# A fused attention and MLP kernel: the next batch's token mix among the last down-products, mixed blocks among the first up-products, and a new order of work in the first phase

## The chip, the core and the metric

One core of a Trainium2 chip. The time is the device time of one launch in microseconds (us), lower is better. All arithmetic is in 32-bit floats; products of the dense layers are made from three passes over split operands (a rounded high part and the rest).

## The reference

Three stages, applied to 4 batches of 768 tokens. A gated linear attention with 8 heads of 48 channels, a token-mixing and channel-mixing layer, and a second one with a spatial gate:

```python
for t in range(S):                                    # attention, per batch and head
    state = alpha[:, :, t, :, None] * state + einsum('bhd,bhe->bhde', k[:, :, t], v[:, :, t])
    y[:, :, t] = einsum('bhd,bhde->bhe', q[:, :, t], state)
...
u = x + (x^T @ U @ V)^T                               # U 768x32, V 32x768: token mix
x = u + relu(u @ w_ch1) @ w_ch2                       # w_ch1 384x1536, w_ch2 1536x384
...
h = relu(x @ w_in); u, v = halves of h                # then layer norm of v, w_spatial over tokens,
out = (u * (w_spatial @ norm(v) + b)) @ w_out         # gate, w_out
```

## The kernel before

Work is written out per engine and ordered by hand; semaphores carry every dependence. TensorE is PE, VectorE DVE, ScalarE ACT, GpSimd POOL, and SP issues all DMAs.

**Attention of a batch** handles the heads in two groups (g = 0, 1) of four. The recurrence over 768 tokens is cut into chunks of 128, and a chunk into levels n = 0 to 7 of blocks that double in size. In a level PE makes scores from the spread queries `Qd` and the keys `K` (L709, L757, L769); ACT `spread`s the next level's queries out of `Q` (L992); DVE takes the wanted part of the scores (`take`, a copy under a mask, L1269) and scales half of the keys by running products of alpha (`scale_k`, L1249); half of the queries is scaled by POOL (`scale_q`, L622) or, in batch 0, partly by DVE (`first_queries`, L1305). The running products are `totals` (L1256), seven small multiplications, each on the result of the one before. Then come the turned keys `kT` (T step, PE L784, copied by DVE in `key_copies` L1332 for group 0), the states (KV step, L797, DVE L1386/L1389), the products with A (AV step, L814) and with the states (Y step, L823), copied by ACT into `xn` (L1099).

**Batch 0** runs its attention alone, the two groups side by side (group 1 uses a second workspace, names with `_side`, and the PSUM banks ZB and HB that the dense layers use later). That is the first 65 us.

**The first dense layer** then runs over a list of units, `UNITS1`: `xu` is the token mix (PE L846, then ACT and DVE split its result into `xu_sb`, L1125 and L1422), `u` 0 to 5 are mixed blocks of 128 channels by 384 tokens (three transposes of `xn`, L861, and one product with V, L877; ACT writes `uh`, L1131, DVE `ul`, L1428), `h` 0 to 23 are up-products (nine matmuls, L832; ACT `hid_hi`, DVE `hid_lo`, L1432), `z` 0 to 23 are down-products (nine matmuls, L909 to L911). `h` runs two units ahead of `z`. The two HB banks alternate over the up-products, the three ZB banks collect the down-products of a half. `UB` names the bank of each mixed block. At the end of a half DVE adds the residual (L1442). The attention steps of the next batch are dealt among the units by `step_slots`, which places them by the units' estimated times. So batches 1 to 3 have their attention under the dense layer of the batch in front.

**Weights.** w1 (six pieces, n = 0 to 5) and w2 (six more) are split into a high part by ACT (`split_high`) and a low part. The low parts of w1 are DVE's (`LOW1`, L1340), those of w2 POOL's (L630/L632 for the first three pieces, `split_low` L639 after). POOL starts on w2 when all six low parts of w1 are there. `split_v` (L1406 to L1414) splits the small matrix V on DVE.

After batch 3 the second dense layer runs for all batches (from about 470 us on); the change does not touch it.

## Time and profile before

| | |
|---|---|
| median of 3 runs | 751.29 us (748.86 to 752.21) |
| profiled execution | 749.4 us, span 747.6 us |
| TensorE busy | 711.8 us, 95% of the span |
| VectorE busy | 346.3 us, 46% |
| ScalarE busy | 327.8 us, 44% |
| GpSimd busy | 202.6 us, 27% |
| DMA | 47.12 MB, mean 63 GB/s |

The span runs from the first to the last instruction of the profiled execution; its own time is 1.8 us longer. A share of busy time is a mean over the whole span, and the first 80 us differ from the rest. Idle time of an engine that nobody waits for costs nothing.

### The profile page before, as it was taken

How to read it: one execution, taken by the hardware profiler on the slowest of the kernel's cores; microseconds unless marked ns; L12 is line 12 of the kernel's file. 1: busy time of each engine (PE TensorE's matmuls, PEld its weight loads, DVE VectorE, ACT ScalarE, POOL GpSimd, SP SyncE). 2: the span in 40 equal slices, each digit the busy share in tenths (PEclk: the TensorE clock that was granted, in tenths of full speed). 3: DMA queues.
4: the chain of work that ended last, by engine and by line, in shares of the span. 5: the costliest groups of instructions: out<-in, count | busy, mean ns of one | idle time of the engine just before them, and what ended most of it. 6: DMA issues, size and time to landing. Idle time of an engine off the chain costs nothing.

```text
span 747.6 us, 25682 instructions
## 1 busy us (share of the span) xinstructions
PE 711.8 (95%) x11408; PEld 673.2 (90%) x11408; DVE 346.3 (46%) x612; ACT 327.8 (44%) x570; POOL 202.6 (27%) x142
## 2 busy tenths in 40 slices
PE   1688899999999999999999999999999999999998
PEld 1578798999898999999999899999999998999998
DVE  5888664645654644764552412116315323431531
ACT  4887446454636445536434322225134232432412
POOL 5404480310450310350220422231330250132031
PEclk9779999999999999999999999999999999999999
DMA  9514501320401220401000332140021002001001
GB/s 290 185 41 139 166 5 38 110 65 8 141 7 35 78 87 17 141 3 41 34 4 3 96 127 63 54 147 12 1 71 57 1 33 95 0 0 63 0 0 63
DMA packets 15693, 47.12 MB, mean 63 GB/s; under 512 B 1681, under 2 KB 8081, under 8 KB 15089
## 3 DMA queue, kind: packets, MB, share of 16 engines
q1 hardware_dynamic: 15600, 45.73, 19.0%
q8 instruction: 77, 1.26, 0.7%
q14 instruction: 16, 0.12, 0.1%
HBM read 36.29 MB, written 9.44 MB: 61 GB/s over the span
## 4 chain that ended last, share of the span: by engine, by line
PE 89%; DVE 4%; issue 1%; ACT 1%; DVEq 0%
PE HB L832 26%; PE ZB L832 9%; PE ZB L909 7%; PE ZB L911 7%; PE ZB L910 7%; PE SB L832 6%; PE SB L709 4%; PE ZB L945 3%; PE HB L945 3%; PE SB L814 2%; PE SB L945 2%; PE SB L823 2%; PE HB L950 2%; PE ZB L950 2%; PE SB L769 1%
## 5 line engine op out<-in xcount | busy, mean ns | idle before, releaser
L1432 DVE SCALAR_TENSOR_TENSOR hid_lo<-HB,hid_hi 128x384 fp32r<-128x384 f32 x96 | 53.4, 557 | 145.0 <-ACT hid_hi L1137 144.2
L1137 ACT ACTIVATE hid_hi<-HB 128x384 fp32r<-128x384 f32 x96 | 47.2, 492 | 157.7 <-PE HB L832 157.5
L832 PE MATMUL HB<-uh,w1h 128*128 128x384 f32 x288 | 103.2, 358 | 2.6 <-DVE ul L1428 1.5
L909 PE MATMUL ZB<-hid_hi,w2h 128*128 128x384 f32 x288 | 98.6, 342 | 0.0
L832 PE MATMUL HB<-ul,w1h 128*128 128x384 f32 x288 | 96.9, 336 | 0.0
L911 PE MATMUL ZB<-hid_lo,w2h 128*128 128x384 f32 x288 | 96.7, 336 | 0.0
L832 PE MATMUL HB<-uh,w1l 128*128 128x384 f32 x288 | 96.6, 335 | 0.0
L910 PE MATMUL ZB<-hid_hi,w2l 128*128 128x384 f32 x288 | 96.3, 334 | 0.0
L662 POOL TENSOR_TENSOR gl<-gated,gh 128x384 fp32r<-128x384 f32 x32 | 32.5, 1015 | 179.6 <-ACT gh L1152 179.6
L992 ACT COPY Qd<-Q 48x768 f32<-48x768 f32 x84 | 73.0, 869 | 14.7 <-PE SB L709 5.7
L622 POOL TENSOR_TENSOR Q<-Q,bk 112x768 f32<-112x768 f32 x13 | 24.8, 1909 | 175.8 <-ACT Qd L992 175.8
L709 PEld LDWEIGHTS SB<-Qd,K 112*32 112x32 f32 x4032 | 41.4, 115 | 26.4 <-issue 16.9
L709 PE MATMUL SB<-Qd,K 112*32 112x32 f32 x4032 | 46.1, 204 | 17.2 <-DMA K<-in_k 10.2
L832 PEld LDWEIGHTS HB<-uh,w1h 128*128 128x128 f32 x288 | 54.0, 187 | 6.6 <-issue 1.4
L622 POOL TENSOR_TENSOR Q<-Q,small 112x768 f32<-112x768 f32 x26 | 42.1, 1618 | 65.6 <-PE SB L757 30.5
L1249 DVE TENSOR_TENSOR K<-K,small 112x768 f32<-112x768 f32 x26 | 47.6, 1829 | 16.9 <-PE SB L769 9.6
L909 PEld LDWEIGHTS ZB<-hid_hi,w2h 128*128 128x128 f32 x288 | 54.0, 188 | 1.1
L832 PEld LDWEIGHTS HB<-uh,w1l 128*128 128x128 f32 x288 | 54.2, 188 | 0.0
L910 PEld LDWEIGHTS ZB<-hid_hi,w2l 128*128 128x128 f32 x288 | 54.1, 188 | 0.0
L832 PEld LDWEIGHTS HB<-ul,w1h 128*128 128x128 f32 x288 | 54.0, 188 | 0.0
L911 PEld LDWEIGHTS ZB<-hid_lo,w2h 128*128 128x128 f32 x288 | 54.0, 188 | 0.0
L1152 ACT CAST gh<-gated 128x384 fp32r<-128x384 f32 x32 | 16.4, 514 | 81.7 <-DVE gated L1478 81.7
(232 smaller groups left out, 1468.6 us busy)
## 6 DMA issues: line engine op xcount, KB each, us to landing
Q<-in_q SPq DMA_DIRECT2D x8, 672.0 KB, 6.5
AL<-in_al SPq DMA_DIRECT2D x7, 672.0 KB, 4.5
K<-in_k SPq DMA_DIRECT2D x7, 672.0 KB, 4.7
Vt<-in_v SPq DMA_DIRECT2D x8, 576.0 KB, 4.0
mid<-x2s SPq DMA_DIRECT2D x8, 576.0 KB, 4.2
x<-mid SPq DMA_DIRECT2D x4, 1152.0 KB, 5.8
out<-o_sb SPq DMA_DIRECT2D x24, 192.0 KB, 1.8
x2s<-in_w SPq DMA_DIRECT2D x9, 384.0 KB, 5.5
```

The lines of the kernel that those rows point to most:

```text
L622: nc.gpsimd.tensor_tensor(qq, qq, t.broadcast_to([ROWS, FLAT // (2 * L), L]), ALU.mult).then_inc(q_ready[g], 1)
L662: nc.gpsimd.tensor_tensor(gl[:, f, t], gated[:, m % 2, :], gh[:, f, t].bitcast(F32), ALU.subtract).then_inc(gl_done, 1)
L709: last = nc.tensor.matmul(bank[j * BLOCK:(j + 1) * BLOCK, u * BLOCK:(u + 1) * BLOCK], keys[:, first_key:first_key + BLOCK], queries[:, u, ...
L832: last = nc.tensor.matmul(dst, weights(x, w), moving(y, m), start=(n == 0 and x == y == 0), stop=(n == total - 1 and y == 1))
L909: nc.tensor.matmul(bank, w2h[:, i, cols], hi, start=(i == 0), stop=False)
L910: nc.tensor.matmul(bank, w2l[:, i, cols], hi, start=False, stop=False)
L911: nc.tensor.matmul(bank, w2h[:, i, cols], lo, start=False, stop=(i == F1B - 1)).then_inc(z_done, 1)
L945: nc.tensor.matmul(bank[:, 0:TH], vh[:, s, i * P:(i + 1) * P], w[:, s, th], start=(s == 0 and w is wsh), stop=False)
L992: nc.scalar.copy(space(a, g).Qd[0 if first else n % 2][r, :, hh, :].rearrange("p u (n l) -> p u n l", l=block_size(n)), targets(Q[g][r, :] ...
L1137: nc.scalar.activation(hid_hi[:, i % HID, :], HB[i % 2][:, 0:TILE], ACT.Relu).then_inc(h_hi, 1)
L1249: nc.vector.tensor_tensor(kk, kk, t.broadcast_to([ROWS, FLAT // (2 * L), L]), ALU.mult).then_inc(k_ready[g], 1)
L1432: nc.vector.scalar_tensor_tensor(hid_lo[:, i % HID, :], HB[i % 2][:, 0:TILE], 0.0, hid_hi[:, i % HID, :].bitcast(F32), ALU.max, ALU.subtra ...
```

## The change

It has four parts.

1. The list of units: four mixed blocks in front of the first up-product instead of six; block 4 behind h 0 and block 5 behind h 1; the token mix of batch b + 1 in front of the last down-product (z 23) of batch b (batch 0's stands alone ahead of the list). `UB` gives blocks 0 and 1 the HB banks, the others the ZB banks. `up` no longer waits for blocks 4 and 5. Since the units' times sit elsewhere in the list, attention steps of the next batch move by up to a unit.
2. The six low parts of w1 go from DVE to POOL, which starts them when DVE has scaled the last queries of batch 0 (`q_ready[1]` at 7); w2's first pieces come behind them.
3. DVE, batch 0: the query scalings of level 2 move up, three of group 1's totals move from level 1 to behind level 2; the copies `A<-Ad` (`square_copies`) are taken apart and moved behind the last key scalings; the V split moves from the T and KV steps to behind all of the attention; the seven totals of batch 1 (`att_start(1, 0)`) move from behind block 5 to ahead of the token mix's low part.
4. SP: the queries of batch 1, group 0 are loaded ahead of the first w2 pieces. ACT: the spreads of level 1 of batch 1 are cut in two, behind h 0 and h 1.

```diff
 def first_units():
-    units = [("xu", 0, NT * NBLK * 2 * 25)]
-    units += [("u", i, 260 + TILE // P * 96) for i in range(NU)]
+    units = [("u", i, 260 + TILE // P * 96) for i in range(DB + 1)]
     for f in range(NF + LAG):
         if f < NF:
             units.append(("h", f, 3 * DB * 173))
+        if DB + 1 + f < NU:
+            units.append(("u", DB + 1 + f, 260 + TILE // P * 96))
+        if f == NF + LAG - 1:
+            units.append(("xu", 0, NT * NBLK * 2 * 25))
         if f >= LAG:
             units.append(("z", f - LAG, 3 * DB * 173))
...
-LOW1 = {(1, KV_STEP): [0, 1, 2, 3], (1, AV_STEP + 1): [4], (1, AV_STEP + 2): [5]}
-SPLIT_V = {(1, LEVELS - 1): [0], (0, T_STEP): [1], (1, KV_STEP): [2]}
...
-        UB = ZB + HB + ZB[:1]
+        UB = HB[::-1] + ZB + ZB[:1]
...
+            load_queries(1, 0, False)
+            sp.wait_ge(ld_q[0], 32)
             for n in range(W1_PIECES, W1_PIECES + STAGE):
                 load_piece(n)
-            load_queries(1, 0, False)
-            sp.wait_ge(ld_q[0], 32)
...
-            pool.wait_ge(w_lo, W1_PIECES)
+            pool.wait_ge(q_ready[GROUPS - 1], LEVELS - 1)
+            for n in range(W1_PIECES):
+                split_low(n)
             for n in range(W1_PIECES, W1_PIECES + STAGE):
                 split(n)
...
 def up(b, f):
-                if f < 2:
-                    pe.wait_ge(u_lo, NU * b + DB + 1 + f)
-                else:
+                if f >= 2:
                     pe.wait_ge(h_lo, NF * b + f - 1)
...
             for n in range(1, MASKED):
                 for g in range(GROUPS):
-                    if (g, n) == (0, 2):
-                        first_queries(0, n)
                     for piece in range(vector_pieces(n)):
                         att_piece(0, g, n, piece, True)
-                    if (g, n) == (0, 1):
+                    if g == 0 and n in (1, 2):
+                        first_queries(n - 1, 2)
+                    if (g, n) == (1, 2):
                         totals(0, 1, range(4, LEVELS - 1))
...
-                if (g, n) == (1, MASKED):
-                    for h in range(GROUPS):
-                        square_copies(h, QUARTERS[2:])
+                if (g, n) == (0, LEVELS - 1):
+                    square_copies(0, QUARTERS[2:])
                 if (g, n) == (0, T_STEP):
                     key_copies(g)
+                    square_copies(1, QUARTERS[2:])
...
-                for m in LOW1.get((g, n), []):
-                    split_low(m)
-                for part in SPLIT_V.get((g, n), []):
-                    split_v(part)
-
+            for part in range(3):
+                split_v(part)
+            att_start(1, 0)
+
+            mix_low(0)
```

DVE in levels 1 to 3 of batch 0; `Ad<-masks` is a take, `small_side` a total of group 1, and the program's tile numbers stand behind Q (69 is group 0, 71 group 1). Before:

```order
L1256 TENSOR_TENSOR small_side<-small_side 112x48
L1256 TENSOR_TENSOR small_side<-small_side 112x24
L1256 TENSOR_TENSOR small_side<-small_side 112x12
L1269 COPY_PREDICATED Ad_side<-masks,ZB 128x384
L1305 TENSOR_TENSOR Q_69<-Q_69,bk 112x384x2
L1269 COPY_PREDICATED Ad<-masks,SB 128x192x2
L1305 TENSOR_TENSOR Q_71<-Q_71,bk_side 112x384x2
L1249 TENSOR_TENSOR K<-K,bk 112x384x2
L1269 COPY_PREDICATED Ad_side<-masks,ZB 128x192x2
L1249 TENSOR_TENSOR K_side<-K_side,bk_side 112x384x2
L1269 COPY_PREDICATED Ad<-masks,SB 128x96x4
```

And with the change, the same stretch:

```order
L1316 TENSOR_TENSOR Q_69<-Q_69,bk 112x384x2
L1280 COPY_PREDICATED Ad_side<-masks,ZB 128x384
L1280 COPY_PREDICATED Ad<-masks,SB 128x192x2
L1260 TENSOR_TENSOR K<-K,bk 112x384x2
L1316 TENSOR_TENSOR Q_71<-Q_71,bk_side 112x384x2
L1280 COPY_PREDICATED Ad_side<-masks,ZB 128x192x2
L1260 TENSOR_TENSOR K_side<-K_side,bk_side 112x384x2
L1267 TENSOR_TENSOR small_side<-small_side 112x48
L1267 TENSOR_TENSOR small_side<-small_side 112x24
L1267 TENSOR_TENSOR small_side<-small_side 112x12
L1280 COPY_PREDICATED Ad<-masks,SB 128x96x4
```

The three totals now stand behind the key scaling of level 2 and directly in front of the take of level 3.

DVE behind the last query scaling of batch 0 (`Q_71<-Q_71,small_side`), with the change; the first row of `xu_sb` is the low part of the token mix:

```order
L1316 TENSOR_TENSOR Q_71<-Q_71,small_side 112x12x64
L1414 CAST V_hi<-V_in 32x384
L1416 TENSOR_TENSOR V_sb<-V_in,V_hi 32x384
L1414 CAST V_hi<-V_in 32x384
L1416 TENSOR_TENSOR V_sb<-V_in,V_hi 32x384
L1408 CAST V_sb<-V_in 64x768
L1267 TENSOR_TENSOR bk<-AL 112x768
L1267 TENSOR_TENSOR bk<-bk 112x384
L1267 TENSOR_TENSOR small<-bk 112x192
L1267 TENSOR_TENSOR small<-small 112x96
L1267 TENSOR_TENSOR small<-small 112x48
```

Two more totals follow, and then the four subtractions `xu_sb<-HB,xu_sb`. Before, the six subtractions `w1l` and the cast of V stood between that query scaling and `xu_sb`, and the totals came behind `ul` of block 5.

DVE at the border between two batches, before; `x2s<-ZB` adds the residual at the end of a half, `xu_sb` belongs to the next batch's token mix, `ul` to its mixed blocks, the take `Ad` and `K` to the attention of the batch after it:

```order
L1442 TENSOR_TENSOR x2s<-ZB,x2s 128x384 x3
L1422 TENSOR_TENSOR xu_sb<-HB,xu_sb 32x96 x4
L1269 COPY_PREDICATED Ad<-masks,SB 128x384
L1249 TENSOR_TENSOR K<-K,AL 112x768
L1428 TENSOR_TENSOR ul<-ZB,uh 128x384 x3
L1428 TENSOR_TENSOR ul<-HB,uh 128x384 x2
L1428 TENSOR_TENSOR ul<-ZB,uh 128x384
```

And with the change; `hid_lo` is the low part of an up-product:

```order
L1423 TENSOR_TENSOR xu_sb<-HB,xu_sb 32x96 x4
L1448 TENSOR_TENSOR x2s<-ZB,x2s 128x384 x3
L1434 TENSOR_TENSOR ul<-HB,uh 128x384 x2
L1280 COPY_PREDICATED Ad<-masks,SB 128x384
L1260 TENSOR_TENSOR K<-K,AL 112x768
L1434 TENSOR_TENSOR ul<-ZB,uh 128x384 x2
L1438 SCALAR_TENSOR_TENSOR hid_lo<-HB,hid_hi 128x384
L1434 TENSOR_TENSOR ul<-ZB,uh 128x384
```

The first up-product of a batch waits for three `ul`; the third of them now has the take and a key scaling in front of it.

## Rows read from the trace of the kernel before

**Rows 1.** The page: busy times, and TensorE's busy tenths in 40 slices

```profile
PE 711.8 (95%) x11408; PEld 673.2 (90%) x11408; DVE 346.3 (46%) x612; ACT 327.8 (44%) x570; POOL 202.6 (27%) x142
...
PE   1688899999999999999999999999999999999998
```

**Rows 2.** Windows: busy us and count of PE, PEld, DVE, ACT, POOL; clock, DMA share, GB/s

```profile
28.00:47.00 19.00, 15.67 (x834) 14.64 (x836) 16.02 (x21) 14.97 (x23) 9.83 (x6) 0.50 0.04 9
...
66.00:81.00 15.00, 11.05 (x259) 9.47 (x250) 12.77 (x24) 10.66 (x20) 7.10 (x6) 1.00 0.65 195
```

**Rows 3.** Timeline of DVE, levels 1 to 3: start us, us, line, operation, idle before

```profile
22.44 0.63 DVE L1256 TENSOR_TENSOR small_side<-small_side 112x48 f32<-112x48 f32 x3 [0.15 <-DVE Ad L1269]
...
29.00 1.17 DVE L1249 TENSOR_TENSOR K_side<-K_side,bk_side 112x768 f32<-112x768 f32 x1 [0.20 <-DVE Ad_side L1269]
30.09 0.58 DVE L1269 COPY_PREDICATED Ad<-masks,SB 128x384 f32<-128x384 uint32 x1
31.28 0.95 DVE L1249 TENSOR_TENSOR K<-K,SB 112x768 f32<-112x768 f32 x1 [0.60 <-issue]
```

**Rows 4.** Timeline of POOL and ACT in the same stretch

```profile
25.32 1.68 ACT L992 COPY Qd<-Q 48x768 f32<-48x768 f32 x2 [1.47 <-DVE Q L1305]
...
27.08 2.27 POOL L622 TENSOR_TENSOR Q<-Q,bk 112x768 f32<-112x768 f32 x1 [15.45 <-ACT Qd L992]
```

**Rows 5.** Timelines of POOL and DVE where both read SBUF together

```profile
71.50 1.84 POOL L632 TENSOR_TENSOR w2l<-x2s,w2h 128x768 fp32r<-128x768 f32 x1
...
71.76 2.39 DVE L1256 TENSOR_TENSOR bk<-AL 112x768 f32<-112x768 f32 x1
...
106.62 3.21 DVE L1249 TENSOR_TENSOR K<-K,small 112x768 f32<-112x768 f32 x1 [1.38 <-PE SB L769]
...
118.06 0.95 DVE L1256 TENSOR_TENSOR bk<-AL 112x768 f32<-112x768 f32 x1
...
120.03 0.93 DVE L1256 TENSOR_TENSOR small<-small 112x96 f32<-112x96 f32 x4
```

**Rows 6.** Timeline of DVE, end of batch 0's attention and token mix

```profile
46.69 1.12 DVE L1398 COPY A_side<-Ad_side 32x768 f32<-32x768 f32 x2
...
49.70 0.35 DVE L1412 CAST V_hi<-V_in 32x384 fp32r<-32x384 f32 x1
...
50.67 1.45 DVE L1332 COPY bk<-SB 128x448 f32<-128x448 f32 x3
...
58.55 0.95 DVE L1305 TENSOR_TENSOR Q<-Q,small_side 112x768 f32<-112x768 f32 x1
59.42 2.69 DVE L1340 TENSOR_TENSOR w1l<-x2s,w1h 128x768 fp32r<-128x768 f32 x3
...
66.64 1.11 DVE L1422 TENSOR_TENSOR xu_sb<-HB,xu_sb 32x96 fp32r<-32x96 f32 x4 [1.47 <-ACT xu_sb L1125]
```

**Rows 7.** Timeline of PE, token mix to the scores of batch 1's level 1

```profile
65.13 1.20 PE L846 MATMUL HB<-xn,U_sb 128*32 128x96 f32 x48 [0.61 <-issue]
...
71.06 0.41 PE L832 MATMUL HB<-uh,w1h 128*128 128x384 f32 x1 [0.76 <-DVE ul L1428]
...
80.11 1.02 PE L709 MATMUL SB<-Qd,K 112*32 112x32 f32 x96 [1.57 <-ACT Qd L992]
```

**Rows 8.** The chain that ended last, one up-product: start us, us, what

```profile
82.89 1.56 PE HB L832 x9
```

**Rows 9.** Timelines at the borders to batches 1 and 3

```profile
184.16 1.60 DVE L1442 TENSOR_TENSOR x2s<-ZB,x2s 128x384 f32<-128x384 f32 x3 [2.63 <-PE ZB L911]
...
185.03 1.20 PE L846 MATMUL HB<-xn,U_sb 128*32 128x96 f32 x48
...
192.00 0.44 PE L832 MATMUL HB<-uh,w1h 128*128 128x384 f32 x1
...
414.27 1.20 PE L846 MATMUL HB<-xn,U_sb 128*32 128x96 f32 x48
...
420.21 0.41 PE L832 MATMUL HB<-uh,w1h 128*128 128x384 f32 x1 [0.76 <-DVE ul L1428]
```

More of the change, by code:

```diff
@@ L865, in mixed @@
                 t, d = divmod(i, DB)
+                if b == 0 and i == 0:
+                    for k in (0, *range(2, 2 + DB)):
+                        turned(b, k)
+                elif b or i in (1, NU - 1):
+                    turned(b, i)
                 if i == 0:
-                    for k in range(DB):
-                        turned(b, k)
                     pe.wait_ge(xu_hi, XU_HI * (b + 1))
@@ L872, in mixed @@
                         pe.wait_ge(v_split, 3)
-                elif i >= DB:
-                    turned(b, i)
                 pe.wait_ge(xu_lo, NBLK * b + (d * P + P - 1) // XW + 1)
@@ L987, in _, with spread @@
         def _(act):
-            def spread(a, g, n, first):
-                for hh in range(2):
+            def spread(a, g, n, first, parts=range(2)):
+                for hh in parts:
                     r = slice(hh * ROW1, hh * ROW1 + HD)
@@ L1006, in att_start, with att_second @@
                 spread(a, g, 0, first)
-            def att_second(a, g):
+            def att_second(a, g, parts=range(2)):
                 pa, pg = before(a, g)
@@ L1013, in att_second @@
                     act.wait_ge(zeroed_q[0], 2)
-                spread(a, g, 1, False)
+                spread(a, g, 1, False, parts)
             def first_spread(g, n):
@@ L1366, in att_piece @@
                     dve.wait_ge(tot_ready[g], R + n - 1)
-                    if first and n == 2 and g == 0:
-                        first_queries(1, n)
                     scale_k(a, g, n)
@@ L1537, in _ @@
                     low(b, kind, i)
-                    if b == 0 and (kind, i) == ("u", NU - 1):
-                        att_start(1, 0)
             for j in range(TWO.n):
```

57 lines of the change are left out of this document (33 added, 24 removed).

## The prediction, made before the changed kernel ran

> **What bounds the kernel now.** I read the page first: TensorE is busy 95% of the span, and its busy tenths are at 9 from about the fifth slice on; only the first four slices, 75 us, show gaps [rows 1]. Then windows: between 66 and 81 us TensorE works 11.05 of 15 us [rows 2]. So from about 81 us on TensorE sets the pace and the change can only win or lose there what it makes TensorE wait; ahead of that a chain through DVE, ACT and PE sets it, and each microsecond added to or taken from that chain moves everything behind it. I read it in the timelines of DVE [rows 3, 6], POOL and ACT [rows 4, 5] and PE [rows 7], and last the borders between batches [rows 9].
>
> **One behaviour decides the sum.** DVE and POOL stand in each other's way when both read SBUF. The first total of batch 1 takes 0.95 us alone; issued at 71.76, under a POOL subtraction that ran from 71.50 to 73.34, it took 2.39 and ended at 74.15, 0.81 us behind the POOL operation's end [rows 5]. The same at 29.00: a POOL scaling ended at 27.08 + 2.27 = 29.35 [rows 4], the DVE key scaling issued at 29.00 ended at 30.17, 0.82 later [rows 3]. So the DVE operation does nothing until POOL's is over. At 106.62 it took 3.21 us [rows 5]: a waiting DVE operation can even lose the port to POOL's next one.
>
> **Term 1, totals of group 1 ahead of level 3: +4.0 us.** Before, the three totals ran at 22.44 in 0.63 us, with POOL idle until 27.08 [rows 3, 4]. Now they stand between the level 2 key scaling and the level 3 take. The query scaling moves up, so ACT's spread of level 3 (1.68 us, started at 25.32 when DVE's query scaling released it) starts about 1.4 us earlier, and with it POOL's scaling at about 25.7, which runs 1.5 us (2.27 less what it waited for DVE, an estimate) [rows 4]. Behind it DVE does the key scaling of group 0 (to 28.0), the query scaling of group 1 (28.9), a take (29.9), the key scaling of group 1 (about 31.0; before 30.17 [rows 3]). By then ACT has spread group 1's queries (28.9 + 1.7) and POOL waits for the port: it runs 31.0 to 32.6. The first total comes at 32.6; it releases the port for 0.1 us, and POOL's next scaling, ready since 32.4, runs to 34.3; then the second and third total. The take starts at 34.6, not at 30.09: +4.5, less the 0.5 us gap in front of the next key scaling [rows 3] that need not come again. Bounds: +1.1 if the totals never wait (31.0 + 0.63), +6 if a third POOL scaling gets between.
>
> **Term 2, less on the chain to the states: -1.35 us.** The V pair (49.70 to 50.67, 0.97 us) stands directly ahead of the copies of the turned keys, and the second `A_side` copy pair (1.12 us) ahead of the last key scaling [rows 6]. The first goes wholly; of the second about 0.4 us counts, since scores of the last level would have held the key scaling anyway. The cover is that DVE's copies now fit while PE turns the keys. Bounds: -0.9 and -2.1.
>
> **Term 3, POOL's low parts of w1 against the token mix: +8.7 us.** Removed from DVE: six subtractions, 2.69 us for three [rows 6], so 5.4 us. Added to POOL: six of 1.84 us, as its w2 subtraction of the same 128x768 [rows 5], 11.0 us. They start when DVE ends the last query scaling, 59.50 [rows 6] less term 2, 58.15. From there DVE has the V split (0.35 + 0.55, twice, and a cast of about the same: 2.5 us) and the seven totals (118.06 to 120.96, 2.9 us [rows 5]); alone it would be done at 63.6, ahead of the token mix's low part, which starts at 66.64 - 1.35 = 65.3 [rows 6]. But nine of these twelve operations read two SBUF operands, and nearly each has to wait for a semaphore of the one before, a gap in which the waiting POOL operation takes the port. I let all six POOL subtractions get in between: 58.15 + 5.4 + 6 x 1.84 = 74.6, less about 0.6 us of starting time hidden in the waits, 74.0. Then the four subtractions of the token mix, which read PSUM (1.11 us [rows 6]): 75.1 where 66.4 was due. Queued behind them on DVE are all `ul`, and so every up-product. This is the largest and least certain term. Bounds: 0 (DVE keeps the port from one short operation to the next) and +13.4 (the three w2 pieces, their transfers issued around 66 us, get in too: three times 2.6 us, less those for which the data comes late).
>
> A rule of the Trainium skill bears on this. SBUF — State Buffer, section Who interferes with whom, says that the port pair shared by VectorE and GpSimd is an exclusive lock held for a whole instruction, taken by whoever issues first, that VectorE needs it with two SBUF inputs or in a two-port mode (casts), and that subtractions from PSUM do not. The trace agrees for the long ones (2.39 against 0.95 us); no row here shows it for operations of 0.2 us. By that rule term 3 would be at its upper end, by a view in which the ports only share bandwidth at about +2.
>
> **Term 4, what comes behind the token mix of batch 0: -1.6 us.** Now: token mix at 65.13, h 0 at 71.06 after 0.76 us of waiting for a `ul`, scores of level 1 at 80.11 after 1.57 us of waiting [rows 7], and only then z 0. With the change the totals no longer stand between the `ul` and h 0's low part, but the chain to the level 1 scores (blocks 0 to 3, h 0, second half of the spread behind h 1, block 5, two query scalings, a take and a key scaling on DVE) stays about as long, 12.4 us from the low part's end; PE does z 0 in it, nine matmuls of 1.56 us in all [rows 8]. Bounds: 0 and -3.
>
> **Term 5, the borders to batches 1, 2 and 3: +1.7 us.** Before, from the token mix to h 0: 192.00 - 185.03 = 6.97 us at the first border, 420.21 - 414.27 = 5.94 at the last [rows 9]. With the change z 23 (1.56 us) covers the splitting of the token mix. But h 0 waits for the third `ul`, and DVE now has in front of it: low part 1.1 (till 1.6 us behind the mix's end), the residual additions 1.6 [rows 9], two `ul` 1.0, a take and a key scaling 2.0, the `ul` 0.5: 6.7 us, when PE has had work for 4.6. h 0 starts 7.75 us behind the mix's start, with blocks 4, 5 and a level of scores (1.95 us) still to do and z 23 (1.56) done: 8.1 against 6.97, +1.1 there and about +1.3 at the second. At the third no attention stands in the way: I get -0.7. Bounds -2 and +3.
>
> I cost at nothing: the earlier load of the queries (they are first needed behind the mixed blocks on ACT; the token mix hides it), and w1's low parts for the up-products themselves: three are done 5.5 us after 58.15, h 0 is far later. The w2 pieces come later on POOL, but z 0 is later still.
>
> **Sum:** 4.0 - 1.35 + 8.7 - 1.6 + 1.7 = +11.45 us on 749.4 us of the profiled execution, 760.9. The median shown is 751.29, 1.9 us above; on its scale I say 762.
>
> **Rivals.**
> - *No change (751 us).* DVE's short operations keep the port, and POOL is the one that waits: term 1 is +1.1, term 3 about 0, the others as above: -0.2. For it: POOL did wait for DVE in places. Against: every DVE operation with two SBUF operands issued under a POOL one waited.
> - *Faster (747 us).* The change does what its order suggests: totals and V split leave the chain and nothing takes their place, terms 1 and 3 nil, the borders gain 0.7 each from the covered splitting: -1.35 - 1.6 - 2.1 = -5. It decides if POOL gets in front of DVE at most once in each of the two places. Against: the same rows.
> - *Strict taking of turns (767 us).* Each DVE operation lets one POOL operation in, w2's too: term 3 is +13.4, sum +16.2.
> - *The clock (767 us).* TensorE waits some 9 us at the token mix. Between 28 and 47 us it ran at a granted clock of 0.50, its 1.2 GHz level, behind a stretch with little work, and between 66 and 81 at 1.00 [rows 2]. If it falls again, 10 us of up-products at half speed cost +5 on top.
>
> **Chances.** My forecast 0.48, strict turns 0.10, clock 0.08, no change 0.22, faster 0.12. The forecast's own range is 757 to 768 (term 1 from +2 to +6, term 3 from +5 to +12). The range for 8 in 10 is 749 to 770: it cuts off the faster case and the ends of the last two. A measurement of this kernel tells about 0.5%, 3.8 us, from no change: faster 0.12, same 0.22, slower 0.66.
>
> **What would show it.** In the timeline of the changed kernel: the take of level 3 near 34 us instead of 30.09; DVE operations of V and totals of 1.5 to 2.5 us between POOL subtractions behind 58 to 62 us; `xu_sb` subtractions of DVE waiting behind a total, with xu's high part done long before; PE idle 5 to 12 us ahead of the first mixed product. If the totals behind the last query scaling take 0.2 to 0.95 us each, term 3 is wrong, and with it most of the forecast. At the borders: PE idle about 2 us ahead of h 0, released by `ul`.

## The result, and the profile after

The changed kernel takes 780.75 us in the median of 4 runs (777.22 to 782.56), the kernel before, beside it, 751.23: a ratio of 1.0395, 95% interval 1.0371 to 1.042. It is slower by 29.5 us. Forecast were 762 us and a range of 749 to 770, so the direction was right and the size too small by 19 us. The profiled execution took 777.2 us, the fastest of the four, with a span of 775.4 us, 27.8 us more than the kernel before. Executions more than 1.5% above the fastest of their kernel count as slow and are left out of the ratios here; only e8 has one (769.47 us).

The page after, the same two parts as in [rows 1]:

```profile
PE 720.4 (93%) x11408; PEld 680.4 (88%) x11408; DVE 356.8 (46%) x606; ACT 328.7 (42%) x570; POOL 212.6 (27%) x148
...
PE   1587689999999999999999999999999999999998
```

TensorE is a little longer busy, and once more it is the first slices that show the gaps: six of 19.4 us, so up to 116 us. (In [rows 1] it is five slices, 93 us, not the four that the forecast read there.) Where the 27.8 us were lost is read from the starts of the four token mixes (PE, `HB<-xn,U_sb`). They are the same landmark in every kernel here, so I list the distances for all of them, with the kernels of the experiments below; numbers in us, worked out from each kernel's timeline of PE and its span. In the new unit order z 23 (1.56 us, [rows 8]) stands behind the mix, so the first distance is shorter by that and the last one longer.

```
kernel           mix 0   0 to 1   1 to 2   2 to 3   3 to end
before           65.13   119.90   115.06   114.18   333.33
after            70.07   136.63   116.66   117.38   334.66
e1_totals_back   65.00   136.69   117.45   117.24   334.62
e2_pool_late     69.66   134.21   122.29*  117.45   334.69
e3_first_only    68.53   131.15   114.57   114.17   333.38
e4_units_only    66.93   123.81   122.17*  117.14   334.65
e5_w1_on_dve     68.75   130.25   123.85*  117.00   334.65
e6_interleave    69.65   137.53   123.39*  117.43   334.60
e7_filled        71.02   134.09   117.25   121.53*  334.71
e8_units_three   68.83   123.46   114.68   115.32   334.61
e9_al_held       69.01   135.92   119.05*  117.58   334.64
e10_mended       66.61   128.02   114.71   115.08   334.68
e11_chain_only   66.74   120.33   114.45   113.95   333.33
* a stop of TensorE in this stretch, see below
```

The column "mix 0" holds one thing that no edit made: group 1's first scores wait for their keys to be loaded, and start at 16.67 us before, 16.82 in the changed kernel, but 18.42 in e4, 19.48 in e8 and 17.59 in e10.

So the changed kernel loses 4.9 us up to the first mix, 16.7 from there to the second (18.3 with z 23 counted), 1.6 and 3.2 in the two next distances.

**Levels 2 and 3 of batch 0**, timeline of VectorE, in place of [rows 3]:

```profile
28.33 0.94 DVE L1316 TENSOR_TENSOR Q<-Q,bk_side 112x768 f32<-112x768 f32 x1
29.20 1.01 DVE L1280 COPY_PREDICATED Ad_side<-masks,ZB 128x384 f32<-128x384 uint32 x1
30.41 0.96 DVE L1260 TENSOR_TENSOR K_side<-K_side,bk_side 112x768 f32<-112x768 f32 x1 [0.20 <-DVE Ad_side L1280]
31.28 3.13 DVE L1267 TENSOR_TENSOR small_side<-small_side 112x48 f32<-112x48 f32 x2
...
34.61 0.56 DVE L1280 COPY_PREDICATED Ad<-masks,SB 128x384 f32<-128x384 uint32 x1
```

and GpSimd in the same stretch:

```profile
31.07 1.80 POOL L623 TENSOR_TENSOR Q<-Q,bk_side 112x768 f32<-112x768 f32 x1 [3.48 <-ACT Qd_side L997]
32.83 1.54 POOL L623 TENSOR_TENSOR Q<-Q,small 112x768 f32<-112x768 f32 x1
```

Three totals that took 0.63 us [rows 3] now end only at 34.61, 0.24 us after the second of two GpSimd (POOL) scalings; the take of level 3 is at 34.61, where the forecast had 34.6. I call this the early jam.

**Between the last query scaling and the token mix's low part**, timeline of VectorE, in place of [rows 6]:

```profile
64.50 0.35 DVE L1414 CAST V_hi<-V_in 32x384 fp32r<-32x384 f32 x1
64.88 2.05 DVE L1416 TENSOR_TENSOR V_sb<-V_in,V_hi 32x384 fp32r<-32x384 f32 x1
67.04 1.78 DVE L1414 CAST V_hi<-V_in 32x384 fp32r<-32x384 f32 x1
68.86 2.05 DVE L1416 TENSOR_TENSOR V_sb<-V_in,V_hi 32x384 fp32r<-32x384 f32 x1
70.94 2.06 DVE L1408 CAST V_sb<-V_in 64x768 fp32r<-64x768 f32 x1
72.92 0.94 DVE L1267 TENSOR_TENSOR bk<-AL 112x768 f32<-112x768 f32 x1
73.90 2.04 DVE L1267 TENSOR_TENSOR bk<-bk 112x384 f32<-112x384 f32 x1
75.97 1.84 DVE L1267 TENSOR_TENSOR small<-bk 112x192 f32<-112x192 f32 x1
77.85 3.54 DVE L1267 TENSOR_TENSOR small<-small 112x96 f32<-112x96 f32 x4
81.42 1.10 DVE L1423 TENSOR_TENSOR xu_sb<-HB,xu_sb 32x96 fp32r<-32x96 f32 x4
```

and of GpSimd:

```profile
64.54 5.95 POOL L640 TENSOR_TENSOR w1l<-x2s,w1h 128x768 fp32r<-128x768 f32 x3 [21.13 <-DVE Q L1316]
70.46 7.14 POOL L640 TENSOR_TENSOR w1l<-early,w1h 128x768 fp32r<-128x768 f32 x3
77.55 0.95 POOL L631 CAST w2h<-x2s 128x768 fp32r<-128x768 f32 x1
78.58 1.80 POOL L633 TENSOR_TENSOR w2l<-x2s,w2h 128x768 fp32r<-128x768 f32 x1
```

The six subtractions of w1 lie in one row without a gap, and VectorE gets one held instruction in for each of them (the cast at 64.50 and the total at 72.92 are not held). Behind them w2's first piece holds the last four totals: the first of them takes 0.76 us beside the cast of w2, the second (78.64) takes 1.80 us and ends 0.06 us after the subtraction of w2. The two shapes of a lost port are to be seen here: a casting instruction of 0.35 us that takes 1.78, and four totals of 0.93 us together [rows 5] that take 3.54. I call this the late jam.

**TensorE behind it**, in place of [rows 7], and windows (columns as in [rows 2]):

```profile
70.07 1.20 PE L850 MATMUL HB<-xn,U_sb 128*32 128x96 f32 x48 [0.61 <-issue]
...
82.09 0.66 PE L882 MATMUL HB<-V_sb,xu_sb 96*128 96x384 f32 x1 [9.36 <-DVE xu_sb L1423]
...
85.52 0.66 PE L835 MATMUL HB<-uh,w1h 128*128 128x384 f32 x1 [1.08 <-DVE ul L1434]
...
97.94 1.02 PE L712 MATMUL SB<-Qd,K 112*32 112x32 f32 x96 [1.36 <-ACT Qd L997]
...
107.37 1.02 PE L712 MATMUL SB<-Qd,K 112*32 112x32 f32 x96 [2.36 <-ACT Qd L997]
```

```profile
48.00:57.00 9.00, 9.00 (x116) 8.72 (x116) 7.36 (x11) 6.85 (x15) 0.00 (x0) 0.50 0.02 5
...
70.00:76.00 6.00, 2.66 (x60) 2.30 (x60) 5.90 (x5) 1.43 (x5) 6.00 (x4) 1.00 0.59 185
76.00:80.00 4.00, 0.00 (x0) 0.00 (x0) 3.93 (x3) 0.00 (x0) 3.92 (x3) 0.73 0.55 209
80.00:90.00 10.00, 6.83 (x21) 6.16 (x22) 4.93 (x12) 4.60 (x8) 5.56 (x5) 0.50 0.64 175
```

A wait of 9.36 us, during which the granted clock falls, and ten microseconds at half clock behind it (1.2 of 2.4 GHz): the products of h 0 stand 0.32 us apart there and 0.17 us before. The wait at 107.37 is put down to ScalarE's `Qd`, which was done at 102.97; what came last is VectorE's key scaling, which met the port again (before, the same scaling took 1.00 us, at 86.38):

```profile
104.22 3.05 DVE L1260 TENSOR_TENSOR K<-K,bk 112x768 f32<-112x768 f32 x1
```

**A wait that the forecast did not have** stands at the products with A, twice in the attention of batch 1 (1.09 us at 139.60, and the first row) and once in that of batches 2 and 3, and one that it had at the borders (timeline of PE, up to the borders to batches 1 and 2):

```profile
193.79 0.89 PE L817 MATMUL SB<-Vt,A 128*32 128x48 f32 x64 [1.23 <-ACT A L1043]
...
214.10 0.45 PE L835 MATMUL HB<-uh,w1h 128*128 128x384 f32 x1 [1.31 <-DVE ul L1434]
...
310.46 0.89 PE L817 MATMUL SB<-Vt,A 128*32 128x48 f32 x64 [1.23 <-ACT A L1043]
...
331.13 0.45 PE L835 MATMUL HB<-uh,w1h 128*128 128x384 f32 x1 [1.68 <-DVE ul L1434]
```

### The profile page after: what moved, and what is told of

It is laid out like the page before. It is cut to its first block, busy times and chain, and to the rows that moved or that the text cites. A ratio compares the mean times of both kernels' runs of the same rounds, so it can differ in the third digit from the quotient of the medians.

```text
span 775.4 us, 25676 instructions
## 1 busy us (share of the span) xinstructions
PE 720.4 (93%) x11408; PEld 680.4 (88%) x11408; DVE 356.8 (46%) x606; ACT 328.7 (42%) x570; POOL 212.6 (27%) x148
## 3 DMA queue, kind: packets, MB, share of 16 engines
q1 hardware_dynamic: 15600, 45.73, 18.3%
## 4 chain that ended last, share of the span: by engine, by line
PE 85%; DVE 6%; ACT 3%; issue 2%; DVEq 0%; ACTq 0%
PE HB L835 25%; PE ZB L835 9%; PE ZB L912 7%; PE ZB L914 6%; PE ZB L913 6%; PE SB L835 6%; PE SB L712 4%; PE ZB L948 3%; PE HB L948 3%; PE SB L948 2%; PE SB L817 2%; ACT A L1043 2%; PE HB L953 2%; PE ZB L953 2%; PE SB L772 2%
## 5 line engine op out<-in xcount | busy, mean ns | idle before, releaser
L912 PE MATMUL ZB<-hid_hi,w2h 128*128 128x384 f32 x288 | 101.7, 353 | 0.3 <-DVE ul L1434 0.3
L1260 DVE TENSOR_TENSOR K<-K,small 112x768 f32<-112x768 f32 x26 | 47.0, 1807 | 13.1 <-PE SB L772 8.5
```

What stands on the lines that cost most here:

```text
L912: nc.tensor.matmul(bank, w2h[:, i, cols], hi, start=(i == 0), stop=False)
L1260: nc.vector.tensor_tensor(kk, kk, t.broadcast_to([ROWS, FLAT // (2 * L), L]), ALU.mult).then_inc(k_ready[g], 1)
```

## The experiments

All are compared with the kernel before on the same chip (medians 750.4 to 751.4 us). None leaves out a part of the computation; e7 does some transposes several times over.

### e1: the three totals back

```diff
-                    if (g, n) == (1, 2):
+                    if (g, n) == (0, 1):
                         totals(0, 1, range(4, LEVELS - 1))
```

> The changed kernel with one thing undone: DVE computes group 1's three last totals between level 1 and level 2 again, where GpSimd is idle. Theory (the SBUF port): the take of level 3 starts near 30.5 us instead of 34.6, everything behind it moves by the same 4 to 4.5 us, and the time falls to about 776.5 us. Rival (the stall ahead of level 3 is only covered slack, and the granted clock sets the first 60 us): the token mix of batch 0 moves by less than 2 us and the time stays within 2 us of 780.7.

777.84 us (772.84 to 782.64), ratio 1.0356 (1.0308 to 1.0404), which overlaps the changed kernel's interval, so the profile has to tell. In the profiled execution the take of level 3 starts at 31.30, the level 3 score at 33.51 in place of 36.79 and the first mix at 65.00 in place of 70.07. The rest is untouched:

```profile
77.01 0.66 PE L882 MATMUL HB<-V_sb,xu_sb 96*128 96x384 f32 x1 [9.35 <-DVE xu_sb L1423]
```

So the three totals are 3.3 us of waiting. Of the 5.1 us at the mix 1.8 more go with TensorE's clock: from the level 3 score to the mix it is 33.28 us in the changed kernel, at half clock from 48 to 57 us as shown above, and 31.49 here at full clock. The last level's scores and the turned keys, which lie there, take 9.24 us (47.88 to 57.12) and 7.58 (44.56 to 52.14). e2, e3, e5, e7 and e9, which have the same early jam, show 31.75 to 32.13 for the stretch; e6, at half clock in the same place (0.52), shows 33.54. e9 is at half clock already from 28 us on, but at full clock again when half of its keys are turned (about 55 us), and takes 31.86. When the clock falls differs between executions with the same jam; what decides it stays open.

### e2: w1's low parts on GpSimd, but later

```diff
-            pool.wait_ge(q_ready[GROUPS - 1], LEVELS - 1)
+            pool.wait_ge(xu_lo, NBLK)
```

> The changed kernel with one wait moved: GpSimd starts the low parts of w1 only when the low part of batch 0's token mix is done, so the V split and the seven totals of DVE run with GpSimd idle. Theory (the SBUF port): DVE's twelve operations take 5.5 us in all instead of 17, TensorE's 9.4 us wait ahead of the first mixed product goes below 1 us; the first up-product then waits for three low parts (5.5 us), so it starts 6 to 8 us earlier than now, and the clock does not fall behind it: 769 to 774 us. Rival (those DVE operations are slow for another reason, such as memory layout or their waits): they stay at 1.5 to 2 us each and the time stays near 781 or grows by the later low parts.

779.84 us (777.39 to 780.92), ratio 1.0369 (1.0319 to 1.042): missed. The late jam was gone (TensorE's wait for `xu_sb` was 0.19 us), but TensorE waited behind it instead:

```profile
77.77 0.69 PE L835 MATMUL HB<-uh,w1h 128*128 128x384 f32 x1 [3.97 <-POOL w1l L640]
...
93.33 1.12 PE L712 MATMUL SB<-Qd,K 112*32 112x32 f32 x96 [4.44 <-ACT Qd L997]
```

At neither of the two places do the eleven microseconds of GpSimd work fit between the attention and h 0: put early they take VectorE's port, put late h 0 needs them, and the port is taken all the same (the second wait stands behind a VectorE query scaling that takes 2.62 us at 86.62 in place of 0.95). The clock falls as well (0.51 from 78 to 84 us), which the theory had ruled out. This run also showed the stop of TensorE told below.

### e3: the first phase alone

The kernel before with parts 2 and 3 of the change and the load order of part 4, and the old unit list.

```diff
-LOW1 = {(1, KV_STEP): [0, 1, 2, 3], (1, AV_STEP + 1): [4], (1, AV_STEP + 2): [5]}
-SPLIT_V = {(1, LEVELS - 1): [0], (0, T_STEP): [1], (1, KV_STEP): [2]}
...
+            pool.wait_ge(q_ready[GROUPS - 1], LEVELS - 1)
+            for n in range(W1_PIECES):
+                split_low(n)
...
+            for part in range(3):
+                split_v(part)
+            att_start(1, 0)
```

> The kernel before with parts 2 to 4 of the change alone (low parts of w1 on GpSimd, new DVE order, earlier query load), the list of units as before. Theory (two port jams, one ahead of level 3 and one ahead of the token mix): it carries the loss of the first 85 us, 14 to 17 us over the kernel before, 765 to 768 us. Rival (the list of units is what costs): within 4 us of 751.

763.84 us (763.19 to 764.19), ratio 1.0164 (1.0118 to 1.0209): 1 us below what the theory expected, and far from the rival's 755. Both jams are there (TensorE waits 3.86 us for the keys of level 3, and 9.67 us in the row below), and behind the second mix nothing is lost (114.57 and 114.17 us between the mixes against 115.06 and 114.18):

```profile
80.53 1.30 PE L877 MATMUL ZB<-V_sb,xu_sb 96*128 96x384 f32 x3 [9.67 <-DVE xu_sb L1419]
```

### e4: the unit order alone

The kernel before with part 1 of the change and ScalarE's half of part 4; the totals of batch 1 follow the fourth mixed block. One line of the edit against the changed kernel, whose other lines put parts 2, 3 and the load order back:

```diff
+                    if b == 0 and (kind, i) == ("u", DB):
+                        att_start(1, 0)
```

> The kernel before with part 1 of the change alone (list of units, banks, token mix inside the down-products, spreads of level 1 cut in two). Theory: it carries what the changed kernel lost behind 98 us, waits of the A products for ACT's square copies (1.2 us, four times) and of the first up-products for DVE (1.3 to 1.7 us, twice) and some in batch 0: 9 to 12 us over the kernel before, 760 to 763 us. Rival (the port jams are all of it, and the list of units costs 2 us as the prediction had it): 752 to 754 us.

766.8 us (761.71 to 767.46), ratio 1.0185 (1.0125 to 1.0244): above the rival and above the theory's 763. The two halves of the change cost 13.1 and 16.1 us in the medians, together 29.2 of the 29.5: they add up. Which half is the larger is not shown, since the unit order's includes the stop told next; the one execution at 761.71 is 11.0 us above the kernel before. Seven of its waits are those of the changed kernel, or near them: 1.09 and three times 1.23 us at the products with A, and 1.30, 1.31, 0.66 at the borders. One is new, and no releaser is shown for it:

```profile
207.94 0.98 PE L712 MATMUL SB<-Qd,K 112*32 112x32 f32 x90
...
212.19 0.26 PE L712 MATMUL SB<-Qd,K 112*32 112x32 f32 x6 [3.27 <-issue]
```

TensorE stops 3.27 us in the middle of one level's scores, with operands there and six products left. Between mixes 1 and 2 it takes 122.17 us, in place of 116.66 in the changed kernel, which has the same program there and no stop. It is the same instruction in e2, e5, e6 and e9 (and its like a batch later in e7), and absent in the profiled execution of the changed kernel. Of e4's four runs three took 766.5 to 767.5 and one 761.7; e3, with the old order, stays within 1 us.

### e5: w1's low parts back on VectorE

```diff
-            pool.wait_ge(q_ready[GROUPS - 1], LEVELS - 1)
-            for n in range(W1_PIECES):
-                split_low(n)
+            pool.wait_ge(w_lo, W1_PIECES)
...
+                for m in LOW1.get((g, n), []):
+                    split_low(m)
```

> The changed kernel with one thing given back: the six low parts of w1 are VectorE's again, at their three old places in batch 0's last attention steps, and GpSimd begins the pieces of w2 once they are done. V's split and the seven totals still stand together ahead of the token mix's low parts. Theory (GpSimd's subtractions take the port between VectorE's dependent instructions): the stretch of casts and totals takes under 5 us in place of 16, TensorE's wait for xu_sb falls from 9.36 to 1 us or less, no stretch at half clock follows, and the kernel takes 766 to 771 us, 10 to 15 below the changed kernel's 780.75. Rival (VectorE simply has too much between the attention and the token mix, whoever holds the port): VectorE has six subtractions more, the wait stays above 5 us, and the time is 778 to 783.

775.31 us (773.88 to 776.33), ratio 1.032 (1.0292 to 1.0349). The mechanism is as the theory has it, the same instructions on VectorE's timeline without GpSimd beside them:

```profile
68.37 0.35 DVE L1419 CAST V_hi<-V_in 32x384 fp32r<-32x384 f32 x1
68.76 0.55 DVE L1421 TENSOR_TENSOR V_sb<-V_in,V_hi 32x384 fp32r<-32x384 f32 x1
...
72.82 0.93 DVE L1266 TENSOR_TENSOR small<-small 112x96 f32<-112x96 f32 x4
```

From V's first cast to the end of the totals it is 5.4 us in place of 16.9. But the six subtractions stand on VectorE ahead of them (5.3 us), so TensorE still waits 3.03 us, and the half clock comes all the same (0.59 and 0.55 from 76 to 84 us). The first distance is 6.4 us shorter and the first mix 1.3 us earlier, and the stop (4.11 us here) takes 7 us back between mixes 1 and 2. The kernel is 5.4 us faster than the changed one, not 10 to 15. The expectation's size was wrong: it left out VectorE's own 5.3 us and took the clock for granted.

### e6: do only dependent instructions lose the port?

In the jam it looked as if each instruction that waits for the result of the one before lets GpSimd in, while the ready one at 72.92 (0.94 us) kept the port. So casts, totals and subtractions were made to take turns.

```diff
-            for part in range(3):
-                split_v(part)
-            att_start(1, 0)
+            mixed_start(1, 0)
...
+                    nc.vector.tensor_copy(V_hi[lo, :], V_in[lo, cols]).then_inc(v_hi, 1)
+                    totals(a, g, [2 * part])
+                    dve.wait_ge(v_hi, part + 1)
```

> The changed kernel; only VectorE's order differs in one stretch: V's two casts and two subtractions and the seven totals of batch 1's group 0 take turns (cast, total, subtraction, total), so that an instruction seldom stands right behind the one whose result it needs. GpSimd's work is untouched. Theory (only an instruction that must wait for its predecessor gives the port away, and a ready one right behind another keeps it): some of the waits of 1.7 us go, TensorE waits for xu_sb 3 to 6 us in place of 9.36, and the time is 770 to 777 us. Rival (GpSimd's waiting subtraction takes the port at every border between two instructions, dependent or not): the same number of waits, 779 to 782 us.

782.87 us (780.78 to 784.79), ratio 1.042 (1.0382 to 1.0457). The theory fell:

```profile
64.09 1.97 DVE L1302 CAST V_hi<-V_in 32x384 fp32r<-32x384 f32 x1
66.10 2.46 DVE L1267 TENSOR_TENSOR bk<-AL 112x768 f32<-112x768 f32 x1
68.59 2.05 DVE L1305 TENSOR_TENSOR V_sb<-V_in,V_hi 32x384 fp32r<-32x384 f32 x1
```

The total at 66.10 does not need the cast before it and still waits. TensorE waits 11.51 us. A waiting GpSimd instruction gets the port at nearly every border of two VectorE instructions; the one at 72.92 is an exception (it stands in e3, e7 and e9 too) whose reason stays open.

### e7: TensorE kept busy in the wait

```diff
-                    for k in (0, *range(2, 2 + DB)):
+                    for k in (0, *range(2, 2 + DB)) * 7:
                         turned(b, k)
```

> The changed kernel, with TensorE's twelve transposes ahead of the first mixed block done seven times in place of once (72 more products of 128 columns, written over each other, some 9 us at full clock), so that TensorE isn't idle while it waits for xu_sb at 71.6 to 82.1 us. Nothing else is touched. Theory (the idle stretch costs twice: the wait, and a stretch at half clock behind it): the granted clock stays at 1.00 from 72 to 92 us, the first up-product of h0 takes about 1.7 us in place of the 3.22 us at half clock, and the kernel ends 3 to 5 us earlier, at 776 to 778 us. Rival (behind the wait the other engines set the pace, so TensorE's clock there costs nothing): 780 to 781 us.

779.71 us (776.6 to 781.32), ratio 1.0376 (1.0337 to 1.0415). Windows:

```profile
76.00:80.00 4.00, 4.00 (x39) 4.00 (x38) 3.90 (x4) 0.00 (x0) 3.92 (x4) 1.00 0.79 293
80.00:84.00 4.00, 2.37 (x20) 1.91 (x18) 3.33 (x7) 0.46 (x1) 3.92 (x3) 1.00 0.38 85
84.00:90.00 6.00, 4.63 (x20) 4.34 (x19) 2.25 (x5) 3.63 (x8) 2.65 (x3) 0.72 0.64 188
```

The clock stays up to 84 us and falls for a part of the next six, after the short waits there. The first distance is 134.09 in place of 136.63 (135.92 in e9 and 136.69 in e1, with the same late jam): so the half clock that the filling took away cost 1.8 to 2.6 us, half of the 5 that the clock rival gave it. The kernel's time misses the expected 776 to 778, and medians 1 us apart don't tell theory from rival here; the distances do.

### e8: the unit order with two places mended

e4's kernel; the last lines shown are VectorE's:

```diff
-                if n == KV_STEP and not first:
-                    square_copies(a, g, QUARTERS)
...
+                if n == T_STEP and not first:
+                    square_copies(a, g, QUARTERS)
...
+                        held = b > 0 and kind == "u" and i < DB + 1
+                        if held:
+                            low(b, kind, i)
```

> The kernel before with the new unit order alone (which took 766.8 us), and two places mended: ScalarE's copies of the level sums that the AV products wait for stand one attention slot earlier (at the T step in place of the KV step), and in the middle batches VectorE takes the second token tile's low parts of the mixed blocks before the attention's pieces that stand in those slots. Theory (the unit order costs what TensorE is seen to wait: 1.09, 1.23, 1.23, 1.23 us at the AV products and 1.3, 1.3, 0.7 us at the borders, and the rest elsewhere): 758 to 761 us, 6 to 9 below. Rival (those waits are slack that comes back at the next one, since the attention's chain sets the pace): 764 to 768 us.

759.16 us (757.8 to 769.47), ratio 1.0106 (1.0069 to 1.0142): as expected, 7.6 under e4. The waits at the products with A are gone from the timeline, those at the first two borders are down to 0.65 us each, and between mixes 1 and 2, and 2 and 3, it takes 114.68 and 115.32 us, about what the kernel before takes. In the first distance only 0.35 us came back: of the waits ahead of the level 1 and level 3 scores (1.40 and 2.07 us in e4) 1.43 and 1.84 are left, and this execution is at half clock for a part of 86 to 90 us (0.60 and 0.55), e4's is not. No stop in the profiled execution; part of the 7.6 us is that, and how much the runs don't tell.

### e9: is the stop a late instruction fetch?

In e5 the load of the decay rows (672 KB) was issued by SyncE 1.6 us ahead of that level's scores (216.50), and one packet of the queue that carries instructions moved in the stop:

```profile
214.87 0.31 SPq L502 DMA_DIRECT2D AL<-in_al  x1
```

```profile
221.59 0.33 PE L711 MATMUL SB<-Qd,K 112*32 112x32 f32 x6 [4.11 <-issue]
```

```diff
+                sp.wait_ge(score_done[0], SCORES * (b + 1) + SCORES - 1)
                 load_decay(b + 1, 1, False)
```

> The changed kernel with one wait added on SyncE: in the middle batches the load of the decay rows (AL, 672 KB) of the next batch's group 1, which stands in the profile right ahead of the level scores at which TensorE was seen to stop for 2.5 to 4.1 us with no releaser shown, is held until group 0's scores are all but one done, some 20 us later; it is needed some 10 us after that. Theory (TensorE's own instructions are fetched behind that load: the stop stands behind the last packets of the load, at the sixth product from the end of a score step that takes 96 products in 1 us; with its stretch at half clock it costs 3 to 5 us, in most runs of the changed kernel, but not in the profiled one): no such stop, and a median of 776 to 778 us with a spread under 2 us, in place of 780.75 (777.22 to 782.56). Rival (the stop has another cause): the same spread of 5 us, and a median of 780 to 781.

778.78 us (777.99 to 783.17), ratio 1.0383 (1.0358 to 1.0408). The load now starts at 241.95. Five of six runs lie within 1.8 us of each other, the median is 2 us lower, but it is above the expected 778, and the stop is still there in the profiled one, shorter:

```profile
224.51 0.26 PE L713 MATMUL SB<-Qd,K 112*32 112x32 f32 x6 [1.37 <-issue]
```

So holding this load doesn't take the stop away. It doesn't leave the place free of loads either: the values (`Vt`, 576 KB) were issued at 216.14, and the last bulk packets are over by 222 us. And the load is not enough for a stop: it is issued 2.7 us ahead of these scores in the changed kernel's profiled execution (221.22 and 223.90), 2.3 in e1 and 1.8 in e8, and none of them stops. So the load can at most lengthen the stop (1.37 us without it, 2.45 to 4.11 with it); the cause stays open.

### e10: everything mended, the unit order kept

The edits of e1, e5, e8 and e9 together on the changed kernel.

> The changed kernel with five places mended at once, its unit order kept: group 1's three totals back behind level 1 (measured -2.9 us), w1's low parts back on VectorE (-5.4 in the medians, -7.7 at the second token mix), ScalarE's copies of the level sums one slot earlier and VectorE's low parts ahead of the attention at a batch's border (-7.6 together), and the decay rows' load held as in the run beside it (-3 to -4). Theory (the costs are separate and add up): 780.75 - 4.5 - 7.7 - 7.4 - 3.5 = 757.7, so 755 to 760 us, still 4 to 10 above the kernel before. Rival (the unit order has a cost of its own that no mended place holds, or the costs hide each other): above 763.

761.39 us (760.73 to 765.06), ratio 1.0149 (1.0125 to 1.0173). Between the theory (755 to 760) and the rival (above 763), and in neither: 19.4 us of the 29.5 come back. What is left stands ahead of mix 1 entirely: mix 0 at 66.61 (+1.5, of which 0.9 is the later landing of group 1's keys), the first distance 128.02 (+8.1, 9.7 with z 23); the other three distances are within 1 us of the kernel before, z 23 counted. Within the first, the timeline of PE:

```profile
72.31 0.66 PE L882 MATMUL HB<-V_sb,xu_sb 96*128 96x384 f32 x1 [3.04 <-DVE xu_sb L1429]
75.73 0.66 PE L835 MATMUL HB<-uh,w1h 128*128 128x384 f32 x1 [1.07 <-DVE ul L1440]
...
97.53 1.02 PE L712 MATMUL SB<-Qd,K 112*32 112x32 f32 x96 [2.35 <-ACT Qd L997]
```

Those are 6.5 us of waiting, where the kernel before waits 0.5, 0.8 and not at all at the same three places: 5.2 of the 9.7. Half clock stands behind the first and the last.

### e11: only the shorter chain

```diff
-                    if (g, n) == (0, 2):
-                        first_queries(0, n)
...
+                    if g == 0 and n in (1, 2):
+                        first_queries(n - 1, 2)
...
+                if (g, n) == (0, LEVELS - 1):
+                    square_copies(0, QUARTERS[2:])
```

> The kernel before with only the part of the change that was to shorten batch 0's attention: VectorE's scalings of the level 2 queries stand up to a step later, the copies of the level sums apart and later. No total, no part of V or w1 and no unit moves. Theory (the gain seen from the first level 3 score to the token mix when the totals were back, 31.49 in place of 32.85 us, is the chain's own): token mix 0 about 1.4 us earlier, and 749 to 750 us, within half a per cent of the kernel before. Rival (the scalings' new place costs at level 2, where a wait of 1.46 us for K_side stands in place of 0.81): 750 to 752.

751.81 us (750.61 to 759.46), ratio 1.0018 (0.999 to 1.0045): no gain, as the rival had it. From the level 3 score to the mix it takes 32.55 us, against 32.85 before; ahead of it `K_side` is waited for longer:

```profile
32.11 1.51 PE L709 MATMUL ZB<-Qd_side,K_side 112*32 112x32 f32 x96 [1.46 <-DVE K_side L1249]
```

where the kernel before waits 0.81 us. The scaling that was moved away from one level stands in the way of another, and the key scaling ahead of it meets GpSimd's scaling (1.71 us at 27.38, in place of 0.94).

## Why the prediction was right or wrong

**Term 1 (+4.0): right, in mechanism and nearly in size.** Two POOL scalings got in between the totals, and the take came at 34.61, reckoned 34.6. From group 1's first score to the level 3 score of group 0 it is 19.97 us in place of 15.61, so +4.4. The totals are 3.3 us of it (e1). The other 1.1 are the moved query scalings: the same stretch is 15.65 us in e4, which has them in the old place, and 16.67 in e1 and 16.71 in e11, which have them in the new place without the jam. The forecast had this inside its chain (the key scaling of group 1 ends at 31.0 in place of 30.17). It took 0.5 us off for a gap in front of the next key scaling, and that gap came again (0.60 us).

**Term 2 (-1.35): not there in the changed kernel.** From the level 3 score to the mix it is 33.28 us against 32.85 before. In the kernels that have the moves and aren't at half clock in the place told under e1 it is 31.5 to 32.3, so 0.5 to 1.4 us were there to win, and TensorE's half clock took them back. The moved scalings and copies alone, with V's split at its old place, give 0.3 (e11, 32.55).

**Term 3 (+8.7): right in kind; nearly in size, and that by some luck.** From the mix's start to the end of the low part was 2.62 us (65.13 to 66.64 + 1.11) and is 12.45 (70.07 to 81.42 + 1.10): +9.8. V's split and the totals take 16.9 us where they take 5.4 when GpSimd is away (e5, and e2 with the same instructions), so they are held for 11.5. Two errors nearly cancel in that. The six subtractions of w1 hold VectorE for 8.9 us, 1.43 to 1.51 each, where the forecast had six times 1.84 less 0.6. And w2's first piece, which it had only in its upper bound, holds the last four totals for 2.6. The token mix's low part, which reads PSUM, was not held (1.10 us beside the next subtraction of w2). The reason given, that a VectorE instruction gives the port away while it waits for the one before, is not the one: in e6 an independent instruction loses it too.

The Trainium skill, SBUF — State Buffer, section Who interferes with whom, has the port pair as an exclusive lock for a whole instruction, to whoever issues first. The trace agrees for 0.35 and 0.55 us instructions too (1.78 and 2.05 us), but not for the total at 72.92, which ran at its own 0.94 us though a GpSimd subtraction had been issued at 72.55. That it is GpSimd's work beside them, and not the instructions themselves, e5 and e2 show; that what they share is the port and not something else is the Trainium skill's account, which every row here fits but that one.

**Term 4 (-1.6): wrong, it was a loss of 1.5.** From the low part's end to the level 1 scores the forecast kept the 12.4 us of before (67.75 to 80.11), with z 0's 1.56 us done inside at no cost. It is 15.4 us (82.52 to 97.94). The step that failed is that z 0 fits in for nothing, and most of it is TensorE's clock: the stretch begins at half clock (0.50 from 80 to 90 us). At full clock it takes 13.36 us in e4, and 13.61 in e7, where it is down for a shorter time; that would have been a gain of 0.6 or 0.3. I had the clock as a rival with a chance of 0.08 and at 5 us, though my own forecast contained the 9 us of idling ahead of it; e7 prices it at 1.8 to 2.6.

**What was not looked at: the level 1 scores to mix 1. This step failed most plainly.** The prediction went from the level 1 scores straight to the border and put the stretch between at nothing. There 108.76 us pass in place of 104.92, and z 0 and z 23 no longer lie in it (3.1), so 7.0 us are lost. TensorE waits 5.66 us there in place of 0.99: 2.36 behind the key scaling that meets the port at 104.22, 1.09 and 1.23 at the products with A, 0.68 for another key scaling, 0.30 for a spread; and it is at half clock from 109 to 112 us. The unit order alone does it: in e4, without the late jam, the stretch takes 107.84 us, 6.0 of the 7.0. The port clash is of the kind that [rows 5] showed at 106.62, where it cost nothing because TensorE was ahead by other work.

**Term 5 (+1.7): right for the borders, and blind for the batches between.** From mix to h 0 it is 7.40 us at the first border, reckoned 7.75; by the forecast's own sum (h 0's start, plus 1.95 still to do, less z 23) that is +0.8, reckoned +1.1. In the same way the second is +1.6, reckoned +1.3 (7.77 us in place of 6.60), and the third -0.9, reckoned -0.7 (5.63 in place of 5.94, with only blocks 4 and 5, 1.0 us, still to do). That makes +1.5, with the waits for `ul` where they were said to be. But the shift of the attention by half a unit put ScalarE's copies of the level sums behind an up-product's high part, and the products with A wait for them, 1.09 to 1.23 us four times; two of these lie behind mix 1. e8 shows that it is these copies' place: with them a slot earlier, and `ul` ahead of the attention, the waits at A are gone and the middle batches take within about 1 us of what they took before. "Attention steps move by up to a unit" stood in the description of the change; I priced only the borders. It is the same omission as in the stretch ahead of mix 1.

**The stop of TensorE** goes with 2.4 to 7 us where it stands (119.05 to 123.85 us between mixes 1 and 2 in place of 116.66). It isn't in the 27.8 us of the profiled execution. That it is why the changed kernel's median lies 3.5 us above its profiled run is likely, from the two levels of e4's times, and not shown.

**The sum.** Of the 27.8 us of span, with z 0 and z 23 counted where they were done: 4.9 up to mix 0 (reckoned 2.65), 9.8 for the late jam (8.7), 1.5 from there to the level 1 scores (-1.6), 7.0 from these to mix 1 (nothing), 4.6 behind it (1.7). Of the 16 us that were missing, 7.0 lie in the stretch that the sum left out, 3.1 in term 4, 2.9 behind mix 1, 2.3 ahead of mix 0 (1.8 of them term 2) and 1.1 in term 3. The sum itself has a slip that changes nothing: 760.9 and 1.9 are 763, not 762.

## What to carry to other kernels

When a change shifts a whole stream of work by half a unit, walk through one full period of it on every engine, not only its borders: small waits within the periods here outweighed what the borders cost. A move away from one place is priced at both ends, and a long wait of TensorE is charged with the half clock behind it. Here a queue of GpSimd instructions of 1.84 us that read SBUF cost nearly each short VectorE instruction about 1.5 us, so such a queue belongs where VectorE works from PSUM or idles.

## What the runs showed of the hardware that was not expected

- The port goes to the waiting GpSimd instruction at nearly every border of two VectorE instructions, dependent or not (e6; 2.46 us for an independent total in place of 0.94), and casts of 32 rows are held too (1.97 us in place of 0.35).
- TensorE stopped for 1.37 to 4.11 us within a run of small matmuls, always behind the 90th or 91st of 96 in one level's scores, with no releaser, in the profiled executions of six of the ten kernels with the new unit order; in the three with the old order the longest pause within a level's scores is 0.23 us (e11), though e3 has one of 1.49 us without a releaser ahead of a level's scores (at 114.92). A bulk load in front of it goes with the longer ones, and stands ahead of the same scores without a stop in three others. Its cause is open.
- After TensorE had been idle for 9.36 us it ran at half clock until about 91 us, 9 us after work came back; with the same wait filled (e7) it was at full clock up to 84 us. After the stop of 4.11 us in e5 it was at half clock from 222 to 226 us.
